# Expert layer with skipped tiles: skips counted at once on the matmul engine, the first layer's values handed on by halves, and a last expert that scatters only real tiles

## What is computed

```
x = attention(q, k, v) with 4 sink columns and a window of 128   # 2 x 8 heads, 768 rows, 64
x = prelu(x @ w_in, alpha) @ w_out                               # 1536 x 512, hidden 2048
e = argmax(x @ w_gate); keep the first 384 tokens of each e      # 8 experts
out[i] = gate[i] * (relu(x[i] @ w1[e]) @ w2[e]), 0 if not kept   # w1: 512 x 1024, w2: 1024 x 512
```

## Time and profile before

| | us |
|---|---|
| median of 3 runs | 665.7 (664.93 to 667.71) |
| the profiled execution's own time | 666.0 |
| its span, first to last instruction | 664.2 |
| expert stage in the span, from the first gather | 430.2 to 664.2 |
| PE busy | 603.7 (91%) |

### The profile page before, as it was taken

One profiled execution on the slowest core, in us unless ns is written; L12 is line 12 of the kernel. 1 busy time (PEld: TensorE's weight loads), 2 busy tenths in 40 slices (PEclk: granted clock), 3 DMA queues, 4 the chain that ended last, 5 costly groups with the idle time before them and its releaser, 6 DMA issues.

```text
span 664.2 us, 11593 instructions
## 1 busy us (share of the span) xinstructions
PE 603.7 (91%) x3901; PEld 509.9 (77%) x3901; DVE 353.5 (53%) x1035; ACT 282.9 (43%) x681; POOL 144.5 (22%) x188
## 2 busy tenths in 40 slices
PE   7779899999999999999999999988998797769973
PEld 6567788888888888888888999866886576548862
DVE  4668676565556555655554454647174464457010
ACT  5655555333434243334332211347265465448210
POOL 4332222221112222222230000031111142142011
PEclk9989899999999999999999999799999799769997
DMA  6534341101243130201001300269083684683000
GB/s 176 145 80 140 99 128 40 42 17 35 65 111 94 52 79 1 48 14 36 1 17 55 137 1 0 88 226 368 34 301 98 225 287 138 218 295 117 16 21 15
DMA packets 73396, 67.41 MB, mean 101 GB/s; under 512 B 43012, under 2 KB 49172, under 8 KB 73328
## 3 DMA queue, kind: packets, MB, share of 16 engines
q1 hardware_dynamic: 69488, 57.76, 28.1%
q0 software_dynamic: 3840, 8.77, 4.1%
HBM read 57.75 MB, written 12.58 MB: 106 GB/s over the span
## 4 chain that ended last, share of the span: by engine, by line
PE 74%; issue 6%; PEld 5%; ACT 5%; DVE 4%; DMA 2%; ACTq 1%; PEldq 1%; POOL 1%; SPq 0%; DVEq 0%; POOLq 0%
PE bank L884 19%; PE bank L886 18%; PE bank L885 18%; PE bank L874 9%; PE bank L924 4%; PE bank L952 4%; ACT wh L669 2%; PE bank L1018 2%; PEld bank L884 2%; PEld bank L886 1%; PEld bank L885 1%; DVE wl L1184 1%; PEldq L648 1%; DMA fw<-y_scratch,mask 1%; ACTq L648 1%
## 5 line engine op out<-in xcount | busy, mean ns | idle before, releaser
L884 PE MATMUL bank<-wh,rw 128*128 128x512 f32 x416 | 171.2, 412 | 27.2 <-ACTq L648 19.1
L886 PE MATMUL bank<-wh,rw 128*128 128x512 f32 x416 | 166.0, 399 | 0.0
L885 PE MATMUL bank<-wl,rw 128*128 128x512 f32 x416 | 166.0, 399 | 0.0
L884 PEld LDWEIGHTS bank<-wh,rw 128*128 128x128 f32 x416 | 80.3, 193 | 44.2 <-issue 24.7
L884 PE MATMUL bank<-rw,wh 128*128 128x256 f32 x384 | 113.2, 295 | 0.3 <-DVE rw L1260 0.3
L886 PE MATMUL bank<-rw,wl 128*128 128x256 f32 x384 | 108.7, 283 | 0.0
L885 PE MATMUL bank<-rw,wh 128*128 128x256 f32 x384 | 108.5, 283 | 0.0
L784 ACT CAST rw<-fw 128x256 fp32r<-128x256 f32 x96 | 39.0, 406 | 145.7 <-DVE fw L1378 145.3
L886 PEld LDWEIGHTS bank<-wh,rw 128*128 128x128 f32 x416 | 80.1, 192 | 18.0
L1184 DVE TENSOR_TENSOR wl<-fw,wh 128x512 fp32r<-128x512 f32 x136 | 86.2, 685 | 12.6 <-ACT wh L669 10.6
L568 POOL TENSOR_SCALAR fw<-fw,rinv 128x256 f32<-128x256 f32 (+1 forms) x88 | 77.1, 887 | 71.8 <-DVE rinv L1239 71.7
(11 more groups left out here) (113 smaller groups left out, 649.2 us busy)
## 6 DMA issues: line engine op xcount, KB each, us to landing
fw<-in_moe_w_dram SPq DMA_DIRECT2D x104, 256.0 KB
v_raw<-in_moe_w_dram SPq DMA_DIRECT2D x24, 256.0 KB
fw<-in_moe_w_in_dram SPq DMA_DIRECT2D x16, 256.0 KB, 3.5
fw<-in_moe_w_out_dram SPq DMA_DIRECT2D x16, 256.0 KB, 2.7
o_sb<-in_q_dram SPq DMA_DIRECT2D x12, 256.0 KB, 3.3
o_sb<-in_k_dram SPq DMA_DIRECT2D x12, 256.0 KB, 4.3
y_scratch<-fw SPq DMA_DIRECT2D x12, 256.0 KB, 2.1
out_dram<-v_or_route SPq DMA_DIRECT2D x12, 256.0 KB, 3.4
```

Source lines behind the costliest of these rows:

```text
L884: pe.matmul(dst, ah, bh, start=start, stop=False, skip_group_check=True)
L885: pe.matmul(dst, ah, bl, start=False, stop=False, skip_group_check=True)
L886: return pe.matmul(dst, al, bh, start=False, stop=stop, skip_group_check=True)
```

## The change

1. **Skipped items counted at once.** `more_than` is gone. Each engine has, per expert, one If on "more than one tile" with everything of tiles 2 and 3 inside, and one Else in which both skipped items are counted together, by 2 (or 4). In ACT's and DVE's Else this stands ahead of the next expert's w2 pieces, which are written out in both arms.
2. **Transposes as counts.** In the skip arms PE does not drain: a transpose of the identity (`skip`) adds the count. `last_of` still drains, once.
3. **By halves.** `relu`, `hidden_high`, `hidden_low` and `hidden_T` count each half of 512 columns; `hidden_T` and `expert_out` wait for halves. `expert_in` of the next item still waits for both.
4. **Order.** The first tile of the next expert is gathered, transposed and split ahead of this expert's second tile; on PE both stand behind `expert_in` (for expert 0 between its halves). ACT's `relu` of a second tile stands behind 5 of the next expert's pieces, where all of them (14 at expert 0, 8 later) were ahead of it.
5. **The last expert.** PE does `keep_busy(10)` ahead of the last `expert_out`. POOL loads the last expert's count and scatters only tiles that exist.

```diff
-            X_ORDER += [TPE * e + 1] + [TPE * (e + 1)] * (e + 1 < E) + list(range(TPE * e + 2, TPE * (e + 1)))
+            X_ORDER += [TPE * (e + 1)] * (e + 1 < E) + list(range(TPE * e + 1, TPE * (e + 1)))
...
+            def over(self, e, j):
+                return self.eng.If(self.count[e] > j * P)
+            def mark(self, done, n):
+                self.eng.drain().then_inc(done, n)
...
+            gather_to(NA)
+            busy = Busy(pool, (E - 1,))
+            scatter(last)
+            with busy.over(E - 1, 1):
+                scatter(last + 1)
+                with busy.over(E - 1, 2):
+                    scatter(last + 2)
+                    all_scattered(last + 2)
+                all_scattered(last + 1)
+            all_scattered(last - 1)
+            all_scattered(last)
...
                 hidden_high(first)
-                busy.more_than(e, 2, lambda: x_high(first + 2), slot_x_high_split)
-                some(NF2 if e else 2 * NF2 - 2, e + 1)
-                for j in range(1, TPE):
-                    busy.more_than(e, j, lambda: another(j), expert_relu_done, expert_hidden_high_split)
+                with busy.over(e, 1):
+                    with busy.over(e, 2):
+                        x_high(first + 2)
+                    with act.Else():
+                        busy.mark(slot_x_high_split, 1)
+                    some(split, split + 5, e + 1)
+                    relu(first + 1)
+                    some(split + 5, W2, e + 1)
+                    scaled(first)
+                    hidden_high(first + 1)
+                    with busy.over(e, 2):
+                        relu(first + 2)
+                        scaled(first + 1)
+                        hidden_high(first + 2)
+                    with act.Else():
+                        busy.mark(expert_relu_done, 2)
+                        busy.mark(expert_hidden_high_split, 2)
+                with act.Else():
+                    busy.mark(slot_x_high_split, 2)
+                    busy.mark(expert_relu_done, 4)
+                    busy.mark(expert_hidden_high_split, 4)
+                    some(split, W2, e + 1)
...
             def hidden_T(i):
-                pe.wait_ge(expert_relu_done, i + 1)
-                if i:
-                    pe.wait_ge(expert_hidden_low_split, i)
-                for f in range(NF2):
-                    r = tr(HT_BANK[f // 4][:, (f % 4) * P:(f % 4 + 1) * P], h_sb[:, f * P:(f + 1) * P])
-                r.then_inc(expert_hidden_transposed, 1)
+                for c in range(2):
+                    pe.wait_ge(expert_relu_done, 2 * i + c + 1)
+                    if i:
+                        pe.wait_ge(expert_hidden_low_split, 2 * i)
+                    for f in range(NF2 // 2):
+                        fs = slice((NF2 // 2 * c + f) * P, (NF2 // 2 * c + f + 1) * P)
+                        r = tr(HT_BANK[c][:, f * P:(f + 1) * P], h_sb[:, fs])
+                    r.then_inc(expert_hidden_transposed, 1)
...
+            def skip(done, n):
+                tr(H_BANK[0][:, 0:P], ident[:, :]).then_inc(done, n)
...
                 hidden_T(first)
-                busy.more_than(e, 2, lambda: slot_T(first + 2), slot_x_transposed)
-                for j in range(1, TPE):
-                    busy.more_than(e, j, lambda: another(j), expert_hidden_done, expert_hidden_transposed)
+                with busy.over(e, 1):
+                    with busy.over(e, 2):
+                        slot_T(first + 2)
+                    with pe.Else():
+                        skip(slot_x_transposed, 1)
+                    another(1)
+                    with busy.over(e, 2):
+                        another(2)
+                    with pe.Else():
+                        skip(expert_hidden_done, 1)
+                        skip(expert_hidden_transposed, 2)
+                with pe.Else():
+                    skip(slot_x_transposed, 2)
+                    skip(expert_hidden_done, 2)
+                    skip(expert_hidden_transposed, 4)
+            keep_busy(10, H_BANK[0])
             busy.last_of(E - 1, expert_out, expert_out_done)
```

More of the change, by code:

```diff
@@ L517, in _, with __init__, last_of @@
             sp.wait_ge(output_zeroed, 16 * NT)
+        class Busy:
+            def __init__(self, eng, experts=range(E), between=None):
+                self.eng = eng
+                eng.wait_ge(counts_in_sbuf, 1)
+                self.count = {}
+                for e in experts:
+                    self.count[e] = eng.value_load(counts[0:1, e:e + 1], min_val=0, max_val=N)
+                    if between is not None:
+                        between()
+            def over(self, e, j):
+                return self.eng.If(self.count[e] > j * P)
+            def last_of(self, e, finish, done):
+                i = TPE * e
+                with self.over(e, 1):
+                    with self.over(e, 2):
+                        finish(i + 2)
+                    with self.eng.Else():
+                        finish(i + 1)
+                        self.mark(done, 1)
+                with self.eng.Else():
+                    finish(i)
+                    self.mark(done, 2)
+            def mark(self, done, n):
+                self.eng.drain().then_inc(done, n)
         @block.gpsimd
@@ L597, in gather_to, with scatter @@
                         break
[L599 to L604, removed]
+            def scatter(i):
                 pool.wait_ge(expert_out_scaled, i + 1)
@@ L609, in _, with all_scattered @@
                     bounds_check=N - 1, oob_is_err=False).then_inc(output_scattered[i % 2], 16)
[L610 to L648, removed]
+            def all_scattered(i):
+                pool.wait_ge(output_scattered[i % 2], 16 * (i // 2 + 1))
+            gather_to(GR + 2)
+            pool.wait_ge(output_zeroed, 16 * NT)
+            pool.wait_ge(index_steps, NIX)
+            last = NA - TPE
+            for i in range(last):
+                gather_to(i + 6)
+                scatter(i)
+            gather_to(NA)
[9 more added lines that the diff above has]
+            all_scattered(last)
         def wait_half_free(eng, p):
@@ L1101, in _ @@
             keep_busy(6, H_BANK[0])
-            busy = Busy(pe, lambda: keep_busy(5, H_BANK[0]))
+            busy = Busy(pe, between=lambda: keep_busy(5, H_BANK[0]))
             def slot_T(i):
@@ L1117, in expert_in @@
                 if i:
-                    pe.wait_ge(expert_relu_done, i)
+                    pe.wait_ge(expert_relu_done, 2 * i)
                 for c in halves:
```

130 lines of the change are left out of this document (76 added, 54 removed).

## The result

The changed kernel takes 642.82 us (median of 4 runs, 639.67 to 648.06) where the kernel before takes 665.54 (664.93 to 667.71): ratio 0.966, 95% interval 0.958 to 0.974. It is 22.7 us faster; 646 was forecast, with a range of 634 to 655. The profiled execution is the second fastest of the four, 639.96 us, span 638.2. The scatter of the four, 8 us where the kernel before has 3, is itself something to explain.

A forecast was written before the change was run, and what follows sets the result against it. PE, busy 91% of the span, was taken as the bound, so only less standing and full-clock matmuls could help. Terms a to f sum to 19.4 us off 666.0, less 0.3 for the median: 646 us, range 634 to 655.

The forecast's parts named there:

- a, expert 0's `relu`: Expert 0's second tile: PE no longer stands 2.40 us for a `relu` behind 14 weight pieces; -2.4 us.
- b, drains: Drains between the halves of `expert_in` in four experts, 0.23 us each, replaced by transposes hidden in waits; -0.7 us.
- c, the marks: Ends of one-tile experts 2, 4 and 5: PE idles 3.1 us for a long branch, not 5.97; -8.6 us.
- The lower bound of the gap: Least idle at a one-tile end: 1.24 us, as after a second tile, whose marks already follow `hidden_high` directly.
- d, the clock: First matmuls after those three pauses: slow starts cost 6.5 us, half of it taken as saved; -3.2 us.
- e, the last expert: Before the last `expert_out`: -0.8 us from halves despite a long branch, 1.6 from full clock; together -2.4 us.
- f, the end: Program end: two scatters that write nothing, 1.29 us each, are gone; -2.1 us.
- rival 1: PE's jumps find their code, so c, d, e and f reach their outer bounds: 635 us; chance 0.22.
- Rivals 2 to 4: Weights bind, 653 us (0.12); two code fetches in a row, 670 us (0.03); PE waits for `relu` instead, 661 us (0.05).
- Rival 2: Late weight pieces delay ACT and DVE, so one-tile experts take 18.5 us: 653 us; chance 0.12.

The follow-up runs named there:

- the shift: The changed kernel with 45 transposes in an If never taken, so PE's later code lies 91 instructions further on: 632.20 us, ratio 0.948.
- the faster kernels above: The changed kernel with PE's later code moved by 39 instructions (633.19 us) or 91 (632.20 us), and variants of the latter with single parts undone.
- `relu` late: Against the kernel shifted by 91 instructions, ACT's `relu` of a second tile again behind all the next expert's pieces: 635.58 us, ratio 0.954.
- shift by 193: The changed kernel with 96 transposes in an If never taken, so PE's later code lies 193 instructions further on: 636.87 us, ratio 0.955.
- shift by 39: The changed kernel with 19 transposes in an If never taken, so PE's later code lies 39 instructions further on: 633.19 us, ratio 0.947.

## Why the prediction was right, point by point

The forecast was 19.4 us less for the profiled execution; it lost 26.0 (666.0 to 639.96). The median lost 22.7, because the profiled execution is a lucky one of its kernel.

- **a, expert 0's `relu` (-2.4).** Right: the 2.40 us are gone. Undoing it brought 1.64 us of them back in the execution that was traced.
- **b, drains (-0.7).** Right in kind, and the largest miss in size: with the halves, 3.8 us are gone from these places. Four drains between the halves of `expert_in` make 0.9. The drains ahead of a second tile's `expert_in`, which the term left out, make 1.0 (from `hidden_T`'s start 1.41 and 1.45 us before, 0.90 and 0.93 now). The halves were costed at nothing outside the last tile, and this was **wrong**: "The halves give nothing at any place where 24 matmuls lie between giver and taker". The taker that I left out is the mark. It stands behind `hidden_high`, so an earlier `hidden_high` is an earlier mark, with no matmuls between. After a second tile the gap from the transposes' end to the next `expert_in` fell from 1.24 to 0.95 us, twice. The other 1.3 us are not broken down.
- **c, the marks (-8.6).** The forecast was made for the gap from the transposes' end to `expert_in`. It was 5.97 us three times and is now 4.18, 3.96 and 0.88 us: -8.9. (The idle rows, 3.88, 3.41 and 0.56, leave out the transposes that count, which now stand on this path.) The cause is the one forecast, a long branch in place of ACT, but that the sum agrees to 0.3 us is **luck**. I had expected a long branch at every one-tile end, and a gap of 3.1 us; two ends had one, each with a gap about 1 us longer than that, and two had none. Whether a jump hits is a matter of where the code lies, and I took a mean for all of them. The lower bound of the gap, 1.24 us, was 0.36 too high for the reason under b: it is 0.88.
- **d, the clock (-3.2).** The first 12 matmuls take 4.4 us after expert 2, 4.1 after expert 4 (558.37 to 562.51) and 2.76 after expert 5. That sums to 11.3 against 15.1, -3.7. Taking half came near because two of three ends had a long pause, which is not why I took it.
- **e, the last expert (-2.4).** The jump was short here, so the gap from the transposes' end fell from 3.82 to 1.21 us and the 24 matmuls from 7.35 to 5.7: -4.3, the term's outer bound. The filling has no part in it that the run without it can show.
- **f, the end (-2.1).** From `scaled` to the span's end there were 10.6 us before (653.59 to 664.2) and 8.4 now: -2.2.

In all, the 26.0 us are 6.6 more than forecast: 3.1 by b with the halves, 1.9 by e, 0.5 by d, 0.4 by c and f, and 0.7 because the first `expert_in` of the experts began earlier (437.12 and not 437.86), which is no part of the change that I can name. Of the signs that the prediction named, the branches of 2 to 3 us at all four one-tile ends did not come: there were two, of 4.7 and 4.3 us, and the other two ends looked like rival 1.

Rival 1 ("jumps find their code", 635 us) was half true at the changed kernel, and the shift makes it true: 632.2 us. That lies outside the range of 634 to 655, with nothing changed but where PE's code lies, so the forecast's nearness for this one placement is in part luck. Rivals 2 to 4 did not happen in the changed kernel; ACT and DVE never waited for a piece between 540 and 600 us. Rival 2's late pieces do show at expert 5 in the faster kernels above, at 1 to 3 us and not at its 7.

The rule that the prediction drew on (the Trainium skill, Runtime: NRT & Kernel Launch, Instruction fetch mechanics: two blocks, prefetch in sequence alone, a branch out of them waits) agrees with these runs: a shift of the code changes which branches are long, from 4.74 us to 0.34 at most at expert 2, and each long one ends behind a packet of code. That two blocks are what is held was not measured by itself. The same section's 128 KiB for PE's instructions does not agree: by it the target, about 250 instructions on, would have been there already, and the branches of 4.7 and 4.3 us waited for a packet that began after they did.

## What to carry to other kernels

A runtime branch's price is the code it jumps into. An arm that is never taken moves the rest of the code, at no cost that these runs show. Two or three such shifts tell whether the code's place matters: here they gave 6, 10 and 11 us. A long branch costs nothing where the engine still has work queued. To see whether a wait is one for code, look for a packet in the instruction queue that ends a little over a microsecond before the wait does. A count for work that is skipped belongs ahead of any work that nobody waits for, and it inherits the lateness of whatever stands ahead of it. Where two waits end at the same place, taking one away shows the other: cost the second before promising the first. When two ways of counting are compared, measure from product to product: an idle row shrinks when a dummy transpose fills it, and nothing is gained.

## What the runs showed of the hardware that I had not expected

- PE waits for code without any branch: 2.81 us after the first and 2.45 us after the second matmul behind a jump. The profile puts it down to "issue".
- The end of a code packet and the end of the wait for it lie 1.26 to 1.52 us apart, with the DMA queues nine tenths busy and with nearly empty ones. The length of the branch says less: it was 4.7 and 4.3 us in the changed kernel but 2.80 us in the kernel before (expert 2), with the DMA engines at 0.89, 0.98 and 0.95, and 1.0 to 2.4 us at the last expert with nearly empty queues. What made the first two longer was not found.
- The clock after an idle PE does not follow from the length of that one pause. After 1.95 us (`relu` late, expert 5) and after 2.81 us (shift by 193) it was granted 0.50, the lower of its two levels, 1.2 GHz. After 2.02 us (shift by 39, expert 5) and after 2.40 us (the kernel before, expert 0) it was full. In stretches of 2.7 us from the first matmul after the 2.81, the 1.95 and the 2.02 us:

```profile
513.77:516.50 2.73, 2.73 (x7) 2.15 (x7) 2.54 (x5) 1.07 (x3) 1.50 (x1) 0.50 0.78 176
```

```profile
567.78:570.50 2.72, 2.72 (x7) 2.14 (x8) 2.42 (x5) 2.63 (x6) 2.11 (x3) 0.50 0.72 231
```

```profile
568.30:571.00 2.70, 2.69 (x12) 2.26 (x13) 2.40 (x5) 2.60 (x5) 2.09 (x3) 1.00 0.82 278
```

- A drain on PE with a semaphore costs no more than a transpose that adds the same count where another engine is waited for anyway (gaps of 0.88 and 0.95 us either way), and 0.4 us more between two pieces of PE's own work.
